# Attention and two feed-forward layers on one core: six weight halves and the first down weights are split in the first half of the kernel, layer 2 starts with four of its six feature blocks, and the exponentials are written to PSUM

## Time and profile before

| what | us |
|---|---|
| median of three runs | 1020.92 (1016.9 to 1023.32) |
| profiled execution | 1018.07 |
| its span | 1016.3 |
| PE busy | 958.1 (94%) |
| DVE, ACT, POOL busy | 502.8, 435.9, 458.5 |
| mean granted clock of PE | 0.982 |
| HBM traffic over the span | 218 GB/s |

### The profile page before, as it was taken

The page is one execution under the profiler, slowest core; times in us unless marked ns, Lnnn a source line. Parts: engine busy times, 40 slices in busy tenths (PEclk is TensorE's granted clock), DMA queues, the critical chain, the costliest instruction groups (busy, mean ns, idle before and its releaser), DMA issues.

```text
span 1016.3 us, 19067 instructions
## 1 busy us (share of the span) xinstructions
PE 958.1 (94%) x7806; PEld 886.1 (87%) x7806; DVE 502.8 (49%) x755; ACT 435.9 (43%) x713; POOL 458.5 (45%) x628
## 2 busy tenths in 40 slices
PE   6999999897999999999466999999999999999998
PEld 5999998797989999999466888988889889888897
DVE  4764586878377656740244343354433444332331
ACT  3432343333333334422242454645546555464454
POOL 2669968866176501111889233332432333323321
PEclk9999999999999999999888899999999999999999
DMA  9778999998398927862455544645446344463431
GB/s 359 248 279 277 315 325 381 383 305 347 125 363 295 337 98 270 294 228 86 161 198 187 208 157 166 202 148 209 147 164 236 127 166 140 144 245 117 163 114 62
DMA packets 50327, 223.01 MB, mean 219 GB/s; under 512 B 5952, under 2 KB 10048, under 8 KB 42688
## 3 DMA queue, kind: packets, MB, share of 16 engines
q0 software_dynamic: 31936, 165.17, 46.1%
q1 hardware_dynamic: 18304, 56.63, 15.6%
HBM read 178.00 MB, written 43.78 MB: 218 GB/s over the span
## 4 chain that ended last, share of the span: by engine, by line
PE 81%; POOL 6%; DMA 5%; DVE 4%; issue 3%; ACT 0%; SPq 0%; DVEq 0%; POOLq 0%; ACTq 0%
PE mlp_ps L622 18%; PE mlp_ps L623 17%; PE mlp_ps L624 17%; PE attn_ps L624 3%; PE attn_ps L623 3%; PE attn_ps L622 3%; PE scores_ps L624 3%; PE scores_ps L623 3%; PE scores_ps L622 3%; PE attn_ps L615 2%; DMA wb_scratch<-stage_a 2%; PE trans_ps L624 1%; PE trans_ps L623 1%; PE trans_ps L622 1%; DMA late_raw<-w_in 1%
## 5 line engine op out<-in xcount | busy, mean ns | idle before, releaser
L889 ACT ACTIVATE up_m<-mlp_ps 128x384 f32<-128x384 f32 x293 | 143.5, 490 | 353.9 <-PE mlp_ps L624 322.5
L622 PE MATMUL mlp_ps<-yc,wa 128*128 128x384 f32 x472 | 163.0, 345 | 30.7 <-DMA wb<-wb_scratch 22.4
L623 PE MATMUL mlp_ps<-yc,wa 128*128 128x384 f32 x472 | 160.2, 340 | 0.0
L624 PE MATMUL mlp_ps<-yc,wa 128*128 128x384 f32 x472 | 159.9, 339 | 0.0
L1470 DVE SCALAR_TENSOR_TENSOR ramp<-ramp,up_m 128x768 f32<-128x768 f32 x64 | 63.6, 994 | 136.5 <-ACT ramp L1140 136.5
L503 POOL DMA_DIRECT2D wa<-wa_scratch x59 | 31.8, 539 | 216.4 <-PE mlp_ps L624 212.1
L622 PEld LDWEIGHTS mlp_ps<-yc,wa 128*128 128x128 f32 x472 | 90.0, 191 | 40.9 <-issue 23.3
L622 PE MATMUL mlp_ps<-yc,wb 128*128 128x384 f32 x354 | 119.9, 339 | 1.1 <-DMA wb<-wb_scratch 1.0
L623 PE MATMUL mlp_ps<-yc,wb 128*128 128x384 f32 x354 | 119.2, 337 | 0.0
L624 PE MATMUL mlp_ps<-yc,wb 128*128 128x384 f32 x354 | 118.6, 335 | 0.0
L540 POOL CAST wo<-wo_raw 128x1024 fp32r<-128x1024 f32 x32 | 33.4, 1043 | 178.6 <-PE trans_ps L624 178.6
(11 more groups left out here) (183 smaller groups left out, 2164.8 us busy)
## 6 DMA issues: line engine op xcount, KB each, us to landing
wa<-wa_scratch POOLq DMA_DIRECT2D x59, 1024.0 KB, 5.2
wb<-wb_scratch POOLq DMA_DIRECT2D x59, 768.0 KB, 6.8
qk_raw<-qk_l SPq DMA_DIRECT2D x24, 768.0 KB, 8.2
wo_raw<-w_out POOLq DMA_DIRECT2D x32, 512.0 KB, 4.0
v_raw<-v_l SPq DMA_DIRECT2D x24, 512.0 KB, 6.7
wa_scratch<-stage_a POOLq DMA_DIRECT2D x24, 512.0 KB, 5.5
wb_scratch<-stage_a POOLq DMA_DIRECT2D x24, 384.0 KB, 6.3
y_scratch<-up_m SPq DMA_DIRECT2D x32, 192.0 KB, 1.9
```

The costliest lines, as they stand in the source:

```text
L622: pe.matmul(out_ap, a_hi, b_hi, start=first, stop=False, skip_group_check=beside)
L623: pe.matmul(out_ap, a_lo, b_hi, start=False, stop=False, skip_group_check=beside)
L624: return pe.matmul(out_ap, a_hi, b_lo, start=False, stop=last, skip_group_check=beside)
L889: return act.activation(o, i, ACT.Copy)
```

## The change

1. **Halves 28 to 33** move to the periods g = 16 to 21 of the first half. `LATE` and its buffers go. `LAST_PAIR` becomes 30, so halves 24 to 29 alternate between two slots and 30 to 33 use one. The ACT wait ahead of `yc0` rises to 30 halves with it.
2. **The first down split.** `load_wo(0)` is issued at the end of period g = 23 after a wait for all stored halves, `split_wo(0)` and `load_wo(1)` come at the end of g = 25. The two slots `wo` are two tensors now, and the tensors from `wo_raw` on have other places in SBUF, for which some waits change (`split_wo(1)` and the first `bent` wait for layer 2).
3. **Layer 2** takes its first three products over feature blocks 0 to 3, then the same three over blocks 4 and 5, then the other five whole. The matmuls are the same.
4. **Exponentials** of all groups go to PSUM, over their own scores; DVE sums and scales from there into `prob`. PE's next scores wait for the scaling and not for the subtraction. The wait for an earlier transposition moves from ACT to DVE.

The diff, cut to its core:

```diff
@@ -49,10 +49,11 @@
+L2_AHEAD = 3
-EARLY, AHEAD, LAST_PAIR, LATE = 4, 12, 24, 28
-HALF_IN = {g: AHEAD + g for g in range(LATE - AHEAD)}
-HALVES_IN_L2 = {}
+EARLY, AHEAD, LAST_PAIR, HALVES = 4, 12, 30, 2 * ITEMS
+HALF_IN = {g: AHEAD + g for g in range(HALVES - AHEAD)}
+WO_LOAD, WO_SPLIT = HALVES - AHEAD + 1, HALVES - AHEAD + 3
@@ -138,13 +139,11 @@
+        wo_raw = sbuf(ctx, "wo_raw", [2, DM])
+        wo = [sbuf(ctx, f"wo{i}", [2, 2, DM], F32R) for i in range(2)]
+        g_hl = sbuf(ctx, "g_hl", [2, 2, 2, TU], F32R)
-        g_hl = sbuf(ctx, "g_hl", [2, 2, 2, TU], F32R)
-        wo = sbuf(ctx, "wo", [2, 2, 2, DM], F32R)
-        wo_raw = sbuf(ctx, "wo_raw", [2, DM])
-        late_stage = sbuf(ctx, "late_stage", [W_SUMS // 2 + W_COLS])
-        late_raw = sbuf(ctx, "late_raw", [W_RAW // 2])
@@ -156,14 +155,12 @@
                 return early_sums[:, :], up_m5[:, 0:W_COLS]
-            if n >= LATE:
-                return late_stage[:, 0:W_SUMS // 2], late_stage[:, W_SUMS // 2:]
             start = (1 if n >= LAST_PAIR else n % 2) * (W_SUMS // 2 + W_COLS)
-            if n in (0, EARLY, EARLY + 1, LATE):
+            if n in (0, EARLY, EARLY + 1):
                 return None
@@ -436,14 +443,12 @@
-                return late_raw[:, :] if n >= LATE else w_raw[:, n % 2]
+                return w_raw[:, n % 2]
-                if n > LATE:
-                    pool.wait_ge(w_split, 2 * n)
-                elif n >= 2:
+                if n >= 2:
@@ -490,7 +495,7 @@
-                if n + 2 < LATE:
+                if n + 2 < HALVES:
@@ -504,6 +509,27 @@
+            def load_wo(g):
+                if g == 0:
+                    for w in w_stored:
+                        pool.wait_ge(w, 32 * ITEMS)
+                else:
+                    pool.wait_ge(wo_split, 2 * g)
+                pool.dma_start(wo_raw[:, :, :].rearrange("p f d -> p (f d)"), w_out2[g % PAIRS]).then_inc(wo_raw_in, 16)
+            def split_wo(g):
+                pool.wait_ge(wo_raw_in, 16 * (g + 1))
+                if g == 1:
+                    pool.wait_ge(l2_done, 2 * KD * TILES_S)
+                elif g >= 2:
+                    pool.wait_ge(down_done, SUBS * (g - 1))
+                pool.tensor_copy(wo[g % 2][:, 0], wo_raw[:, :, :]).then_inc(wo_hi_done, 1)
+                pool.wait_ge(wo_hi_done, g + 1)
+                for f in range(2):
+                    pool.tensor_tensor(wo[g % 2][:, 1, f], wo_raw[:, f], wo[g % 2][:, 0, f].bitcast(F32),
+                                       ALU.subtract).then_inc(wo_split, 1)
@@ -524,43 +550,16 @@
                 load_wb(g + 2)
-                if (g + 1) % PAIRS_S == 0:
-                    for n in HALVES_IN_L2.get(g // PAIRS_S, ()):
-                        split_begin(n)
-                        split_end(n)
-            def load_wo(g):
-                pool.dma_start(wo_raw[:, :, :].rearrange("p f d -> p (f d)"), w_out2[g % PAIRS]).then_inc(wo_raw_in, 16)
-            def split_wo(g):
-                pool.wait_ge(wo_raw_in, 16 * (g + 1))
-                if g >= 2:
-                    pool.wait_ge(down_done, SUBS * (g - 1))
-                pool.tensor_copy(wo[:, g % 2, 0], wo_raw[:, :, :]).then_inc(wo_hi_done, 1)
-                pool.wait_ge(wo_hi_done, g + 1)
-                for f in range(2):
-                    pool.tensor_tensor(wo[:, g % 2, 1, f], wo_raw[:, f], wo[:, g % 2, 0, f].bitcast(F32),
-                                       ALU.subtract).then_inc(wo_split, 1)
-            pool.wait_ge(l2_done, 2 * KD * TILES_S)
-            load_wo(0)
-            load_raw(LATE)
+                if g == WO_LOAD:
+                    load_wo(0)
+                if g == WO_SPLIT:
+                    split_wo(0)
+                    load_wo(1)
             for g in range(PERIODS):
-                late = [n for n in (LATE + 2 * g, LATE + 2 * g + 1) if n < 2 * ITEMS]
-                for n in late[0:1]:
-                    split_begin(n)
-                    split_end(n)
-                    load_raw(n + 1)
-                split_wo(g)
-                if g + 1 < PERIODS:
-                    pool.wait_ge(wo_split, 2 * (g + 1))
-                    load_wo(g + 1)
-                for n in late[1:2]:
-                    split_begin(n)
-                    split_end(n)
-                    if n + 1 < 2 * ITEMS:
-                        load_raw(n + 1)
+                if g:
+                    split_wo(g)
+                    if g + 1 < PERIODS:
+                        load_wo(g + 1)
                 if g + 2 < PERIODS:
@@ -572,8 +571,8 @@
-                if not isinstance(n, int) or n >= GPT:
-                    pe.wait_ge(sub_done, n)
+                if n >= GPT:
+                    pe.wait_ge(prob_done, n)
@@ -737,30 +736,41 @@
-            def l2_product(v, x):
+            def l2_blocks(v, x, blocks):
                 reuse = SUBS if v == TILES_S - 1 else 3
-                if x >= reuse:
-                    pe.wait_ge(y_copied, y_before(v) + x - reuse + 1)
-                elif v == TILES_S - 1:
-                    if x == SUBS - 1:
+                if blocks[0] == 0:
+                    if x >= reuse:
+                        pe.wait_ge(y_copied, y_before(v) + x - reuse + 1)
+                    elif v == TILES_S - 1:
+                        if x == SUBS - 1:
+                            pe.wait_ge(summed, 4 * (last_pair + 1))
+                    elif x < 2:
+                        pe.wait_ge(summed, 4 * last_pair + 1 + x)
+                    else:
                         pe.wait_ge(summed, 4 * (last_pair + 1))
-                elif x < 2:
-                    pe.wait_ge(summed, 4 * last_pair + 1 + x)
-                elif x == 2:
-                    pe.wait_ge(summed, 4 * (last_pair + 1))
-                for f in range(KF1):
-                    if x == 0 and f in (0, KF1 - 2):
-                        pe.wait_ge(h2_lo_done, 4 * f0 + (3 if f else 0))
-                    if x == 1 and f == KF1 - 1:
-                        pe.wait_ge(h2_lo_done, 4 * f0 + 4)
+                for f in blocks:
+                    if x == 0 and f == 0:
+                        pe.wait_ge(h2_lo_done, 4 * f0)
+                    if x < 2 and f >= KF1 - 2:
+                        pe.wait_ge(h2_lo_done, 4 * f0 + 2 * (f - KF1 + 2) + x + 1)
                     wc = slice(f * DM + d * P, f * DM + (d + 1) * P)
                                  f == 0, f == KF1 - 1)
-                last.then_inc(l2_done, 1)
+                if blocks[-1] == KF1 - 1:
+                    last.then_inc(l2_done, 1)
+            def layer2_large(v):
+                for x in range(L2_AHEAD):
+                    l2_blocks(v, x, range(KF1 - 2))
+                for x in range(L2_AHEAD):
+                    l2_blocks(v, x, range(KF1 - 2, KF1))
+                for x in range(L2_AHEAD, 2 * KD):
+                    l2_blocks(v, x, range(KF1))
@@ -804,8 +814,7 @@
-                    for x in range(2 * KD):
-                        l2_product(v, x)
+                    layer2_large(v)
@@ -860,8 +869,7 @@
-            for x in range(2 * KD):
-                l2_product(TILES_S - 1, x)
+            layer2_large(TILES_S - 1)
@@ -888,11 +896,10 @@
-            def exponent(n, slot):
+            def exponent(n):
                 act.wait_ge(sub_done, n + 1)
-                if not isinstance(n, int) or n >= 2:
-                    act.wait_ge(trans_done, n - 1)
-                act.activation(prob[:, slot], score_of(n), ACT.Exp, scale=float(D) ** -0.5).then_inc(exp_done, 1)
+                act.activation(exp_of(n), by_bank(n, score_of(n)), ACT.Exp,
+                               scale=float(D) ** -0.5).then_inc(exp_done, 1)
@@ -1130,8 +1137,7 @@
                 else:
-                    for w in w_stored:
-                        act.wait_ge(w, 16 * LATE)
+                    act.wait_ge(l2_done, 2 * KD * TILES_S)
                 act.activation(ramp[:, f], up[:, g % 2, f].rearrange("p t c -> p (t c)"), ACT.Relu, bias=half_col[:, 0:1],
@@ -1144,8 +1150,6 @@
                     act.wait_ge(down_done, SUBS * (g - 1))
-                elif g == 0:
-                    act.wait_ge(l2_done, 2 * KD * TILES_S)
                 copy(g_hl[:, g % 2, 0, f], ramp[:, f]).then_inc(g_hi_done, 1)
@@ -1215,18 +1219,24 @@
-            def softmax_scale(n, slot, e):
+            def softmax_scale(n, slot):
+                e = exp_of(n)
+                pair, rec = row_pair[:, :, 0], row_rec[:, :]
+                if n < GPT:
+                    rec = rec.unsqueeze(2).to_broadcast([P, H, WIN])
+                else:
+                    pair = pair.rearrange("p (r j) -> p r j", r=2)
+                    rec = rec.rearrange("p (r j) -> p r j", r=2).unsqueeze(3).to_broadcast([P, 2, HALF_HEADS, WIN])
                 dve.wait_ge(exp_done, n + 1)
-                dve.tensor_reduce(row_pair[:, :, 0], e, X, ALU.add).then_inc(sum_done, 1)
+                dve.tensor_reduce(pair, e, X, ALU.add).then_inc(sum_done, 1)
```

(27 more changed lines are left out.)

## The result

| kernel | median us | runs | lowest to highest |
|---|---|---|---|
| before | 1018.91 | 4 | 1010.21 to 1023.32 |
| changed | 984.16 | 4 | 983.2 to 984.41 |

The ratio is 0.9667 with a 95% interval of 0.96 to 0.9734. The forecast was 983 us (974 to 996). The profiled execution took 983.97 us, 34.1 less than that of before.

A forecast was written before the change was run, and what follows sets the result against it. PE, busy 958.1 of 1016.3 us, was taken as the bound, with POOL's order holding up the second half's first four periods. Terms summed to -36.2, so 981.9; half of a 2.9 us median offset gave 983 us (974 to 996).

The forecast's parts named there:

- second half's start: First four second-half periods: without late halves in POOL's queue, PE's waits for loads and split go, -36.6 us.
- layer 2's order, with the clock: Layer 2's head: new block order covers both waits for `h_lo`, -4.5 us; low clock behind the first goes, -1.6.
- exponentials: Attention: scaling from PSUM takes 691 ns instead of 802; PE sees part of it, -1.5 us (0 to -3).
- halves 28 and 29, second slot: Tile 1: halves 28 and 29 cost nothing; alternating slots for 24 to 27 remove a `wb` wait, -1.0 us.
- tile 2: Halves 30 to 33 there: DVE slowed beside POOL +1.8 us, late loads +5.6, clock dip behind them +1.6.
- The next wait: Layer 2's head: third product, starting 2 us sooner, needs the tile's last sums; they are done, so no wait.
- the one wait that the scaling ended: Attention: of 2.3 us DVE time saved in scaling, PE sees only its wait of 1.65 us at 186.27.
- POOL's chain: Tile 2, one slot: each half's casts wait for the previous store to land, making weight loads late, +5.6 us.
- 3L - 10.6: Tile 2: PE's loss in us from late loads, L being a store's landing time, taken as 5.4: +5.6.
- DVE's slowing: Tile 2: four halves on POOL slow DVE's maxima by 7.1 us; PE loses +1.8 us (0 to +7.1).
- The rival that DVE's slowing reaches PE in full: Tile 2: all 7.1 us of DVE's slowing come through to PE, +5.3 us, total 988; chance 0.06.
- The clock dip: Tile 2: low granted clock behind PE's waits for late loads, +1.6 us (0 to +4.8).

The follow-up runs named there:

- undo_order: Changed kernel with layer 2 in whole products from the first, as before the change: 989.63 us, ratio 0.9738.
- undo_exp: Changed kernel with the exponentials back in SBUF: 990.08 us, ratio 0.9735.
- only_halves: Moved halves and moved first down split alone; layer 2's order and the exponentials as in the kernel before: 995.84 us, ratio 0.9783.
- undo_wo: Changed kernel with the first down weights loaded and split only after the last layer 2, halves still moved: 981.33 us, ratio 0.9663.
- only_exp: Kernel before with the exponentials in PSUM and nothing else changed: 1012.37 us, ratio 0.9957.
- one_slot: Changed kernel with one staging slot from half 24 on, as the kernel before had it: 978.45 us, ratio 0.963.
- after_again: The changed kernel measured and profiled once more, nothing altered: 983.25 us, ratio 0.9669.
- small_two: Changed kernel with POOL's arithmetic of halves 30 to 33 on one column per block and two staging slots to the end: 977.6 us, ratio 0.9614.
- small_split: Changed kernel with POOL's arithmetic of halves 30 to 33 on one column per block, all DMAs kept: 981.79 us, ratio 0.9669.

## Why the prediction was right

The total was off by 1 us, and the steps by more. Terms, forecast against measured:

| term | forecast | measured | from |
|---|---|---|---|
| second half's start | -36.6 | -35.8 | stages |
| layer 2's order, with the clock | -6.1 | -6.4 | undo_order |
| exponentials | -1.5 | -6.8 | undo_exp |
| halves 28 and 29, second slot | -1.0 | +7.2 | only_halves, tile 1 |
| tile 2 | +9.0 | +6.5 | stages |

With the 1.9 us ahead of tile 0 the measured terms give -33.4, the profiled executions -34.1; parts that were undone from one side interact a little. The two terms from undone parts are differences of medians with intervals of several us.

**Second half.** Right in each step. Period 1 took from 482.09 to 497.79, 15.7 us with its start-up waits where I had 15.3, and then three periods of 15.64. The granted clock of the stage rose from 0.88 to 1.00 (2.4 GHz throughout), which the difference of marks had in it; in the second profile of the same kernel the clock dipped once there and the gain is 34.3. In the sum the moved down split had nothing, and undo_wo bears that out: no gain, and at most 0.9 us of loss.

**Layer 2.** Right in the total. The next wait did not come: the third product's sums were there. It started sooner than I wrote, by about 5 us in tile 0 and not 2, since the wait of 3.12 for `h_lo` had stood ahead of it too. The parts are off: 3.5 us of waits for `h_lo` where I had 4.5, and two dips of the clock, 3.4 us together, where I had one of 1.6 and only one stands behind such a wait. That they add up to the forecast is in part luck.

**Exponentials: mis-sized by 5 us.** The step that failed is letting PE see only the one wait that the scaling ended, 1.65 at 186.27. That wait went as forecast. But other waits of the stretch fell with it, those for DVE's sums in both runs, for `h_lo` in only_exp and for ACT's copies in undo_exp, and in the kernel before a dip of the clock went too: only_exp shows 5.3 us in tile 0, of which the scaling's own wait is 1.7. With the moved halves a second scaling became as slow, 2.18 us in tile 1, which a mean of 802 ns over 21 did not announce. The exponential itself could be left out, as I did: 600 ns into PSUM against 630 into SBUF.

**Tile 1: wrong in sign.** "Add what its other periods have without loss: nothing." Of those nine periods seven had a half beside them, four of these in the single slot, and I read it so that the slot held POOL back and kept their loss small. With two slots and two more halves DVE's maxima in tile 1 got slower; here the kernel before (270 to 355 us), then the changed one (266 to 355):

```profile
L1352 DVE TENSOR_TENSOR up_m<-up_m 128x384 f32<-128x384 f32 x22 | 18.8, 872 | 0.4
```

```profile
L1362 DVE TENSOR_TENSOR up_m<-up_m 128x384 f32<-128x384 f32 x24 | 29.3, 1239 | 0.4
```

That is the slow rate of tile 0 in the earlier trace rows. one_slot brings 3.7 us of the stage back. The other 3.5 of the 7.2 would be the two more halves in g = 16 and 17; no run moved these alone.

**Tile 2: near in size, but not by the way forecast.** POOL's chain ran as I had it: POOL waited before each cast, the landings had a median of 5.8 us, and 3L - 10.6 gives 6.8. What it was to cause did not come. I had about 5 us of PE's waits for `wa` or `wb` in periods 21 to 23, and there were none in this profile and 2.1 us in that of after_again; PE waited 3.6 us for ACT and DVE instead. DVE's slowing, which I priced at 1.8 (4/9 of 4.2 is 1.9) and added, cost no less alone than both did together (7.2 and 6.5) and lay beside the chain: not a sum but nearly a maximum. So the size is in part luck. The rival that DVE's slowing reaches PE in full was nearer on that point than my term. The clock dip came once, 0.87 over 404 to 408 us and 0.70 over the next four, 1.7 us in all where I had 1.6; in after_again there was none, and the stage took 68.3 us all the same.

So two misses of 5 and 8 us and one of 2.5 nearly cancelled; the forecast of the total was better than its parts.

On the two rules of the Trainium skill: that a DVE instruction with two SBUF inputs contends with GpSimd's reads (SBUF — State Buffer, Who interferes with whom), the runs bear out on both sides, 691 ns for the scaling from PSUM in every version and 802 to 958 from SBUF. The Trainium skill's figure of about 358 GB/s between HBM and SBUF (SBUF — State Buffer, Summary: rules for kernel authors) is no bar here, since small_two moved 361 GB/s over tile 2 without one wait of PE for a load.

## What to carry to other kernels

Price a slowed operation by its longest instances and by every wait of the stretch that can grow with it, the low clock behind such waits too. The mean of 802 ns hid one of 2.17 us, and the wait that this one ended was 1.7 of the 5.3 us that left tile 0 with it. When two waits can cover the same stretch, their prices do not add, and removing one alone may show next to nothing: remove both once before calling either innocent. A wait off the critical path may be what keeps two engines from colliding, so look at who runs during it before cutting it. And when stages are cut at an engine's event, compare the work counted in them: a mark that the engine reached late looks like a loss in one stage and a gain in the next.

## What had not been expected of the hardware

With its arithmetic nearly gone, POOL did not run ahead. In small_split the cast that waits for a store came 8.4 us after the store's issue, in the changed kernel 6.0:

```profile
380.04 0.55 POOL L502 DMA_DIRECT2D wb_scratch<-stage_a  x1
...
388.41 0.18 POOL L480 CAST stage_a<-w_raw 128x1 fp32r<-128x1 f32 x1 [5.04 <-DMA wb_scratch<-stage_a]
```

```profile
384.71 0.55 POOL L497 DMA_DIRECT2D wb_scratch<-stage_a  x1
...
390.75 0.61 POOL L477 CAST stage_a<-w_raw 128x512 fp32r<-128x512 f32 x1 [2.29 <-DMA wb_scratch<-stage_a]
```

So a cycle of the single slot stayed at 10.3 us in the mean of three, against 10.7. Later landings took up most of what the engine gave back: the stores to `wb_scratch` landed in a median of 7.8 us against 5.8. With two slots (small_two) their median was 9.2, and nobody was held up. Why the landings came later is not shown.
